# Two first batches of a linear-attention block written straight into place, with their bonus sums on TensorE and their state update deferred

## The reference

```python
# attention: batch 4, heads 8, sequence 768, head_dim 48, all fp32
for t in range(S):
    cur = einsum('bhd,bhe->bhde', u[None] * k[t], v[t])
    y[t] = einsum('bhd,bhde->bhe', r[t], state + cur)
    state = w[None, :, :, None] * state + einsum('bhd,bhe->bhde', k[t], v[t])
x = y as [3072 tokens, 384]
# first MLP (384 -> 2048 -> 384)
h = x @ w_in;  g = h * sigmoid(1.702 * h);   x = g @ w_out
# second MLP, its own weights
h = x @ w_in2; g = h * tanh(softplus(h));    out = g @ w_out2
```

## Time and profile before

| what | value |
|---|---|
| median of 3 runs | 919.5 us (919.02 to 2286.22) |
| the profiled execution's own time | 920.33 us |
| its span, first to last instruction | 918.4 us |
| mean granted TensorE clock | 0.987 |
| PE busy | 896.6 us (98%) |
| DVE, ACT, POOL busy | 335.4, 290.4, 178.9 us |

### The profile page before, as it was taken

One profiled execution on the slowest core, in us unless ns is written; L12 is line 12 of the kernel. 1 busy time (PEld: TensorE's weight loads), 2 busy tenths in 40 slices (PEclk: granted clock), 3 DMA queues, 4 the chain that ended last, 5 costly groups with the idle time before them and its releaser, 6 DMA issues.

```text
span 918.4 us, 12827 instructions
## 1 busy us (share of the span) xinstructions
PE 896.6 (98%) x5126; PEld 748.9 (82%) x5126; DVE 335.4 (37%) x465; ACT 290.4 (32%) x526; POOL 178.9 (19%) x145
## 2 busy tenths in 40 slices
PE   7797999999999999999999999999999999999998
PEld 7697888888888888888888888888888888888886
DVE  6474744543443454335145322122121221222211
ACT  1353223223222322322245532332323322322332
POOL 5585850432325043222000000000000000000000
PEclk9798999999999999999999999999999999999999
DMA  9755320321132032112412000000000000000000
GB/s 212 168 113 115 76 67 16 81 52 45 48 82 61 14 82 52 45 48 51 142 53 86 0 1 0 35 1 1 35 0 1 35 1 1 35 0 1 35 1 34
DMA packets 33289, 44.28 MB, mean 48 GB/s; under 512 B 5712, under 2 KB 27856, under 8 KB 33232
## 3 DMA queue, kind: packets, MB, share of 16 engines
q1 hardware_dynamic: 31312, 42.24, 17.3%
q10 hardware_dynamic: 1920, 1.23, 0.6%
HBM read 36.37 MB, written 4.72 MB: 45 GB/s over the span
## 4 chain that ended last, share of the span: by engine, by line
PE 90%; SPq 4%; DMA 2%; issue 1%; POOL 1%; DVE 1%; ACT 1%; POOLq 0%; DVEq 0%; ACTq 0%
PE h L879 42%; PE acc L906 41%; PE y_bank L821 2%; PE a_bank L805 2%; PE y_bank L833 2%; SPq L337 2%; SPq L333 1%; DMA mid<-in_wts 1%; DMA xs<-xs 1%; PE a_bank L846 1%; POOL win_lo L442 1%; SPq L311 0%; PE y_bank L919 0%; PE acc L919 0%; DMA arena<-in_rk 0%
## 5 line engine op out<-in xcount | busy, mean ns | idle before, releaser
L716 DVE TENSOR_TENSOR g_lo<-act,g_hi 128x512 fp32r<-128x512 f32 (+1 forms) x201 | 180.7, 900 | 512.0 <-ACT g_hi L546 511.8
L879 PE MATMUL h<-xs,win_hi 128*128 128x512 f32 (+1 forms) x1206 | 342.2, 387 | 7.6 <-ACT g_hi L546 3.1
L879 PEld LDWEIGHTS h<-xs,win_hi 128*128 128x128 f32 x1206 | 221.9, 191 | 53.6 <-POOL win_lo L442 5.6
L543 ACT ACTIVATE act<-h 128x512 f32<-128x512 f32 (+1 forms) x201 | 116.3, 578 | 274.2 <-PE h L879 274.0
L546 ACT ACTIVATE g_hi<-h 128x512 fp32r<-128x512 f32 (+1 forms) x201 | 116.4, 579 | 255.5 <-PE acc L906 255.4
L906 PE MATMUL acc<-g_hi,wout_hi 128*128 128x512 f32 (+1 forms) x603 | 168.1, 381 | 0.0
L906 PE MATMUL acc<-g_hi,wout_lo 128*128 128x512 f32 (+1 forms) x603 | 168.1, 381 | 0.0
L906 PE MATMUL acc<-g_lo,wout_hi 128*128 128x512 f32 (+1 forms) x603 | 168.0, 381 | 0.0
L879 PE MATMUL h<-xs,win_lo 128*128 128x512 f32 (+1 forms) x603 | 165.6, 383 | 0.0
L879 PEld LDWEIGHTS h<-xs,win_lo 128*128 128x128 f32 x603 | 112.4, 191 | 22.0
L906 PEld LDWEIGHTS acc<-g_hi,wout_hi 128*128 128x128 f32 x603 | 111.6, 189 | 21.6
(11 more groups left out here) (76 smaller groups left out, 421.6 us busy)
## 6 DMA issues: line engine op xcount, KB each, us to landing
arena<-in_rk SPq DMA_DIRECT2D x48, 192.0 KB, 3.5
arena<-in_wts SPq DMA_DIRECT2D x16, 384.0 KB, 3.6
arena<-in_r SPq DMA_DIRECT2D x24, 192.0 KB, 3.8
arena<-in_k SPq DMA_DIRECT2D x22, 192.0 KB, 3.6
arena<-in_v SPq DMA_DIRECT2D x22, 192.0 KB, 3.7
out<-mid SPq DMA_DIRECT2D x5, 768.0 KB, 3.3
xs<-xs SPq DMA_DIRECT2D x141, 16.0 KB, 1.8
mid<-in_wts SPq DMA_DIRECT2D x1, 1152.0 KB, 7.1
```

Of the source, the lines that this page charges most:

```text
L543: act.activation(act1[:, g % 2, 0:c1 - c0], h_bank[g % 2][:, 0:c1 - c0], GATES[layer])
L716: dve.tensor_tensor(g_lo[:, g % 2, cols], act1[:, g % 2, cols], f32(g_hi[:, g % 2, cols]), ALU.subtract).then_inc(glo_done, 1)
L879: ins = pe.matmul(hb, w[:, f, kd, :], x_part(lo, par, kd)[:, c0:c1], start=i + kd == 0, stop=i == 2 and kd == KD - 1)
```

## The change

For the first two batches the two heads of the fourth pair are no longer moved. A copy of their v, split in three pieces of 16 columns each behind 48 columns of zeros (`vs_pad`), is multiplied with their scores over 64 rows, so that the 16-row pieces come out in the rows where the moves would have put them; the other six heads are added on top. The bonus sums of these two batches are made on PE (`early_sums`: the elementwise product of the decayed r and k, times u/w in a small table `pick` loaded one value at a time), so `rr`, the bonus steps and the first reduction fall away for them. Their `ks` are loaded later, and their state update is put at step `LATE` = 8 of the stream. POOL decays `rk` of batch 1 in place of DVE, DVE makes two `low_out`, the loads are put in another order, `HALF` becomes 10, `scores(2)` moves from ahead of the stream into its step 0, and three of the six moves of batch 3 go from SP's queue to ACT's.

```diff
-HALF = 9
+HALF = 10
+LATE = 8
-SCORES = [{2: 3, 8: 4, 12: 5, 15: 6, 18: 7}] + ...
-BURST = [{1: 2, 4: 3, 11: 4, 14: 5, 17: 6, 20: 7}] + ...
+SCORES = [{0: 2, 3: 3, 9: 4, 12: 5, 16: 6, 19: 7}] + ...
+BURST = [{2: 2, 5: 3, 11: 4, 14: 5, 18: 6, 21: 7}] + ...
# SP
-            for n in range(2):
+            for n in range(EARLY):
                 sp.wait_ge(rk_clear, n + 1)
                 load_rk(n)
-                load_kv(n)
-                load_rr(n)
...
+            for n in range(EARLY):
+                load_v(n)
+            sp.wait_ge(cleared, 2)
+            for j, p0 in enumerate((0, ODD)):
+                sp.dma_start(pick[p0:p0 + D, :, j], u_d.rearrange("o (h a d) -> d (o h) a", h=HP, a=2)[:, :, j],
+                             allow_slow_non_contiguous=True).then_inc(pick_in, 16)
+            load_k(2)
+            load_rr(2)
+            for i, (to, rows, landed) in enumerate(pieces):        # group 1
+                if i == 6:
+                    sp.wait_ge(a_done, 2)
+                    sp.wait_ge(prod_done, 1)
+                    load_rk(2)
+                    load_v(2)
                     sp.dma_start(bonus_u, u_d.broadcast_to([P, DM])).then_inc(u_in, 16)
+                sp.dma_start(to, rows).then_inc(landed, 16)
             sp.wait_ge(a_done, 4)
+            sp.wait_ge(prod_done, 2)
             load_rk(3)
+            load_k(3)
             load_rr(3)
-            move_x(0)
-            move_x(1, half=True)
+            sp.wait_ge(dtrn, 1)
             load_group(2)
-            load_again(B)
+            load_v(3)
+            for n in range(EARLY):
+                load_k(n)
             move_x(2)
-            move_x(3)
-            load_again(B + 1)
+            for n in range(B, B + 2):
+                sp.wait_ge(y_done, n - 1)
+                load_rk(n)
+                load_rest(n)
+            move_x(3, half=True)
...
             load_group(3)
             for n in range(B, NT * B):
+                if n + 2 < NT * B:
+                    sp.wait_ge(y_done, n + 1)
+                    load_rk(n + 2)
                 move_x(n)
                 if n + 2 < NT * B:
-                    load_again(n + 2)
+                    load_rest(n + 2)
# GpSimd
+            pool.wait_ge(w_in, 32)
+            pool.wait_ge(pick_in, 32)
+            pool.tensor_tensor(pick, pick, powers[:, 0, 0, :]...broadcast_to([PR_ROWS, HP, 2]), ALU.mult)
             pool.wait_ge(runs, 2 * LOGS)
+            pool.wait_ge(rk_in[1], 32)
+            pool.tensor_tensor(first[1].rk, first[1].rk, decay, ALU.mult).then_inc(r_dec, 1)
+            for n in range(EARLY):
+                product(n)
...
-            for n in range(EARLY):
-                bonus(n)
-            pool.wait_ge(dtab, 1)
-            for n in range(EARLY):
-                decay_k(n)
# ScalarE, ahead of the stream
-            act.wait_ge(kv_in[0], 32)
+            act.wait_ge(rk_in[0], 32)
...
+            for n in range(EARLY):
+                act.wait_ge(v_in[n], 16)
+                act.activation(vs_pad[n][:, :, :, D:ODD], first[n].vs[:, H - 2:H, :]..., ACT.Copy).then_inc(padded, 1)
# ScalarE, in the stream, ahead of the step's split_in and split_out
                     attention(t, s)
+                    if t == 0 and s == LATE:
+                        for n in range(EARLY):
+                            first_state(n)
+                    if t == 0 and s in BURST[t] and BURST[t][s] == B - 1:
+                        act.wait_ge(xlo_done, B)
+                        for i, (to, rows) in enumerate(x_pieces(B - 1)):
+                            if i >= KD:
+                                act.dma_start(to, rows).then_inc(moved[B - 1], 16)
# VectorE, ahead of the stream
             select(0)
-            decay_rk(1)
+            select(1)
             diagonal(0)
-            select(1)
             diagonal(1)
             x_lo_part(0)
             x_lo_part(1)
             decay_rk(2)
-            select(2)
-            diagonal(2)
+            low_out(0)
+            low_out(1)
# TensorE
+                if n < EARLY:                                       # inside(n)
+                    pe.wait_ge(padded, EARLY + n + 1)
+                    for kd in range(KD):
+                        for half, p0 in enumerate((0, ODD)):
+                            pe.matmul(y_of(n)[p0:p0 + ODD, kd * CH:(kd + 1) * CH], vs_pad[n][:, half, kd, :], e.amat[:, half, HP - 1, :],
+                                      start=kd == 0, stop=False, skip_group_check=True)
+                    (six more for heads 0 to 5)
+            def early_sums(n):
+                pe.wait_ge(pick_done, 1)
+                pe.wait_ge(prod_done, n + 1)
+                for hp in range(HP):
+                    ins = pe.matmul(early_dots[n]...[:, hp, :], rk_prod[n][:, hp, :], pick[:, hp, :], start=True, stop=True)
+                if t == 0 and s == LATE:                            # attention(t, s)
+                    pe.wait_ge(state_new, 2 * (B - EARLY))
+                    for n in range(EARLY):
+                        update(n)
             scores(0)
-            decay_rows()
-            keep_warm(early_bank, 6)
-            scores(1)
-            keep_warm(early_bank, 2)
-            inside(0)
-            keep_warm(early_bank, 8)
-            inside(1)
-            update(0)
-            update(1)
-            pe.wait_ge(dtab, 1)
-            keep_warm(decay_bank, 4)
-            scores(2)
-            keep_warm(decay_bank, 8)
+            keep_warm(early_bank, 2)
+            scores(1)
+            early_sums(0)
+            keep_warm(early_bank, 2)
+            early_sums(1)
+            inside(0)
+            keep_warm(early_bank, 2)
+            inside(1)
+            decay_rows()
+            keep_warm(early_bank, 8)
```

More of the change, by code:

```diff
@@ L107, in mlp_rwkv_program @@
         LOGS = CH.bit_length()
+        pick = part(2 * HP)[0:PR_ROWS, :].rearrange("p (h a) -> p h a", h=HP)
         powers = part(LOGS * 2 * HP)[0:PR_ROWS, :].rearrange("p (n s h) -> p n s h", n=LOGS, s=2)
@@ L132, in first_operands, with borrow @@
             return e
+        unused = [(SLOTS - 3) * 2 * DM]
+        def borrow(cols):
+            unused[0] += cols
+            assert unused[0] <= SLOTS * 2 * DM
+            return mid[:, unused[0] - cols:unused[0]]
+        rk_prod = [borrow(HP * CH)[0:PR_ROWS, :].rearrange("p (h t) -> p h t", h=HP) for _ in range(EARLY)]
+        decay_t = borrow(HP * CH)[0:PR_ROWS, :].rearrange("p (h t) -> p h t", h=HP)
+        vs_pad = [borrow(DM).rearrange("p (a k e) -> p a k e", a=2, k=KD) for _ in range(EARLY)]
         later = [operands(b) for b in range(B)]
@@ L151, in mlp_rwkv_program @@
         early_bank = acc[1]
+        early_dots = [bank[:, 0:H] for bank in (y_bank, acc[0])]
         w_in = sem("w_in")
@@ L156, in mlp_rwkv_program @@
         rk_in = [sem(f"rk_in{b}") for b in range(B)]
-        kv_in = [sem(f"kv_in{b}") for b in range(B)]
+        k_in = [sem(f"k_in{b}") for b in range(B)]
+        k_first = [sem(f"k_first{b}") for b in range(EARLY)]
+        v_in = [sem(f"v_in{b}") for b in range(B)]
+        padded = sem("padded")
+        pick_in = sem("pick_in")
+        pick_done = sem("pick_done")
+        prod_done = sem("prod_done")
+        early_done = sem("early_done")
         rr_in = [sem(f"rr_in{b}") for b in range(B)]
@@ L470, in _ @@
                 low_out(f)
+            pool.wait_ge(dtab, 2)
             def low(f0, f1):
@@ L577, in _ @@
             split_out(0, 0)
+            split_out(0, 1)
             split_in(0, 2)
-            act.wait_ge(xlo_done, 2)
-            for i, (to, rows) in enumerate(x_pieces(1)):
-                if i >= KD:
-                    act.dma_start(to, rows).then_inc(moved[1], 16)
-            split_out(0, 1)
-            act.wait_ge(cleared, 2)
-            for n in range(EARLY):
-                first_state(n)
+            act.wait_ge(dtrn, 1)
+            for a, d0 in enumerate((0, ODD)):
+                act.activation(decay_s.rearrange("p (h a d) -> p h a d", h=HP, a=2)[:, :, a],
+                               decay_bank[:, 0:HP * PR_ROWS].rearrange("p (h d) -> p h d", h=HP)[:, :, d0:d0 + D], ACT.Copy).then_inc(dtab, 1)
+            act.wait_ge(cleared, 3)
             gate(0, 0)
@@ L758, in tile @@
                         split_g(g + 1)
-                    if t == 0 and s == 0:
+                    attention(t, s)
+                    if t == 0 and s == 1:
                         decay_rk(3)
-                        dve.wait_ge(dtab, 1)
+                        dve.wait_ge(dtab, 2)
                         decay_k(2)
-                    attention(t, s)
-                    if t == 0 and s == 2:
+                    if t == 0 and s == 4:
                         decay_k(3)
+                    if t == 0 and s == LATE - 1:
+                        for n in range(EARLY):
+                            decay_k(n)
                     if switch:
@@ L848, in update @@
                 ins.then_inc(ds_done, 1)
```

(7 more changed lines are left out.)

198 lines of the change are left out of this document (115 added, 83 removed).

## The result

The median is 908.06 us (907.63 to 909.12, 4 runs) against 919.26 for the kernel before beside it: a ratio of 0.9885, with an interval of 0.9865 to 0.9904. The gain, 1.15%, is clear of the noise and smaller than the 2% that the forecast asked for to call the kernel faster; the forecast's median was 900.6. The profiled execution took 908.21 us, 12.1 less than the one before; 18.9 were forecast.

The account below looks back on a forecast made before the run. PE was taken as busy after 141.64 us, so only the stretch before counted: 33.9 us ahead of the stream, 17.4 lost inside it. Terms summed to -18.9 us, giving 900.6 us; own range 896 to 904, 892 to 910 for 8 in 10.

Parts of the forecast that it names:

- first rival: Prologue slower than worked out: clock falls ahead of `inside(0)`, or `pick` lands late; +3 to +6 us, 905; chance 0.21.
- The new start, -11.8: Ahead of the stream: without moves, tile 0's first `up` comes at 22.1 us, not 33.86, 11.8 us sooner.
- late weights: Rival at the start: weight group 0 lands at 21.70 again, start 23.8, groups 1 and 2 late; 905; chance 0.07.
- slow `pick`: Rival at the start: `pick`'s 384 values served one after another; 909, or 921 and up; chance 0.04.
- The clock at the start: PE's prologue and stream start: clock taken as kept through shorter holes, -2.3 us; if it falls, start some 3.5 later.
- Work inside the stream, +2.6: Tile 0's stream on PE: `scores(2)` 1.28, two late updates 1.1 and the tenth block in halves 0.24 add 2.6 us.
- group 3, -7.8: Weight group 3, issued sooner by SP: ACT's wait, PE's two stalls and the half clock behind them go, 7.8 us less.
- The small waits, -0.5: PE's waits for POOL's `low_in` in the stream: 1.9 us for 2.4, 0.5 us less.
- ACT's moves, +2.2 and +1.9: Step 5: batch 3's moves delay `split_in(8)` and the next step's `up`, +2.2 us; half clock behind the idle time, +1.9.
- The state of piece 5, -3.2: `scores(6)`: `rk` n+2 loaded ahead of the moves of n removes PE's state wait and half clock, 3.2 us less.
- Next late is the same weight group, with two steps of slack on PE: Said of weight group 3: once its wait is gone, the next late thing is that group again, covered by two steps.
- The rival that the moves cost little: DVE or POOL slack swallows ACT's moves of batch 3, or the clock stays up: -4.1 us, 896.5; chance 0.18.

Follow-up runs that it names:

- experiment 6: Changed kernel with all six moves of batch 3 issued by SP, none by ACT: 909.62 us, ratio 0.9884 to the kernel before.
- experiment 8: Changed kernel with low remainders of weight blocks 10 to 15 set to zero by POOL's memset, not subtracted: 906.28 us, ratio 0.9854 to the kernel before.
- experiment 10: Changed kernel with the load of `rk` n+2 behind the moves of n again: 910.9 us, ratio 0.9895 to the kernel before.
- experiment 1: Changed kernel with POOL's wait for `pick` and its product behind the decay of batch 1's `rk`: 907.02 us, ratio 0.9854 to the kernel before.
- experiment 2: Changed kernel with five more `keep_warm` behind `scores(0)` and four ahead of `inside(0)`: 905.68 us, ratio 0.9852 to the kernel before.
- experiment 3: As experiment 2, plus one unused 128-column matmul between each two two-column matmuls of `early_sums`: 908.05 us, ratio 0.9875 to the kernel before.
- experiment 7: Changed kernel with `decay_k(2)` ahead of `decay_rk(3)` on DVE: 908.22 us, ratio 0.9874 to the kernel before.
- experiment 5: Changed kernel with ACT's three moves of batch 3 issued behind the step's splits: 910.0 us, ratio 0.9886 to the kernel before.
- experiment 11: Changed kernel with experiments 2 and 5, and `scores(7)` and the bursts of 5 and 6 one step later: 902.82 us, ratio 0.9817.
- experiment 9: Changed kernel with `select` and `diagonal` ahead of `g_lo` on DVE at tile 0's later steps with `scores`: 909.58 us, ratio 0.9891 to the kernel before.
- experiment 12: Changed kernel with experiments 1, 3 (fewer added warmings) and 5, the steps of experiment 11, late `decay_k` one step sooner: 899.64 us, ratio 0.9795.

## Why the prediction was right or wrong

Right: the direction, and the range (892 to 910, measured 908.06). Too large: the size, 18.9 us for 12.1; the forecast's own narrower range, 896 to 904, was missed. That the wide range held is partly luck: the first rival accounts for 2.6 of the 6.7 us between the two sums, and the other large part, 3.5, is in no rival. The sign "first `up` after 25 us" was missed by 0.4 us, and three of the six other kernels with this prologue show it. Point by point:

- **The new start, -11.8.** `pick`, the weights and `scores(1)` came as worked out, so neither the late weights nor the slow `pick` happened. What failed is the step "*The clock at the start* ... I take it as kept": it kept for the stream (so -2.3 holds) but not for the prologue, where 7 us at half clock cost the start 2.5 (0.7 to 4.2 in the seven kernels with this prologue). That is the first rival. Its reason was half of it: it and the forecast both looked at the holes of PE, and the hole ahead of `scores(1)` does precede the fall in experiments 6, 8 and 10. But experiments 1 and 2 closed the holes to 0.3 to 0.4 us without keeping the clock, and experiment 3 shows that the two-column `early_sums` then bring it down. They had been priced by their time alone (0.5 us).
- **Work inside the stream, +2.6, and group 3, -7.8:** as forecast; the splits that had waited wait 0.31 us in all.
- **The small waits, -0.5, measured +0.7.** The step put the meeting of `decay_rk(3)` with `low_in(4)` on PE's wait for POOL. The wait is on the other side, DVE's `decay_k(2)` behind `decay_rk(3)`, 1.30 us; experiment 7 shows that either order leaves one of the two late.
- **ACT's moves, +2.2 and +1.9:** right in place and size, 2.2 and 1.6. Experiment 5 shows the cause, and also that the loss isn't saved by removing it alone.
- **The state of piece 5, -3.2:** measured -3.5.
- **The missing term, +3.5.** The step that failed is "Next late is the same weight group, with two steps of slack on PE", said of group 3, and with it the step on piece 5, which asked of the sooner loads only what POOL and the state gain. Next late was DVE. PE's stall for group 3 and POOL's pauses had been DVE's time (read from the two timelines; no run puts them back as they were); with them gone or short `g_lo` took 3 us and more beside POOL, and `inside` waited for `diagonal` three times. Experiment 8 shows that POOL's subtractions are behind 0.99 and 1.90 of it, experiment 11 that a step more for DVE ends it. The mechanism was in the earlier trace rows, where `low_in` took 2.42 us; the forecast applied it to step 1 alone.

The rival that the moves cost little didn't happen.

**What stays open.** Which part of the load order takes POOL's pauses, and how much of the 2.9 us is due to POOL's reads rather than to the length of its work. Each term comes from single profiled executions, while the ratios of most experiments overlap: that 1, 2 and 8 are each ahead of the change by some 0.3% isn't settled. Nor is it what decides whether a fall of the clock follows an idle time: behind 2.5 us it did in seven kernels and not in experiment 2, behind the last wait for `diagonal` (1.9 to 1.95 us) it did in experiments 1 and 7 and not in the kernel after.

## What to carry to other kernels

An engine's idle time on a shared resource is another engine's working time: when a load is moved so that one engine no longer waits, look at what its neighbour got done in that pause. Where several waits lie a fraction of a microsecond behind each other, a single repair measures nothing (experiments 5 to 7, 9 and 10 all lie within 0.2% of the change), and only together are they worth their sum (experiments 11 and 12); so after each removed wait ask who is late next, and mend the row of them. Work moved to TensorE in very narrow matmuls is priced by what it does to the clock as well as by its length. And before a cause is read from one trace, look at the same stretch in every kernel that shares it: here seven traces of one prologue showed a fall at three different places.

## What the runs showed of the hardware that was not expected

- Two groups of four two-column matmuls (fp32, so 16 records) are followed by a fall of the granted clock though PE shows as busy: 0.58 over 3.50 us with PE busy for 3.50 (experiment 2), and 1.00 over 4.00 us with a 128-column one between each two (experiment 3).
- A hole of 1.20 to 1.67 us behind `scores(0)` was followed by a fall within `scores(1)` in three kernels, one of 0.96 to 1.17 us in four was not; the falls there came later, at 14 to 16 us.
- The element-wise load of `pick`, 384 values of 4 bytes in two transfers, landed 4.2 us after its issue, and the 192 KB load of v issued just ahead took 4.5. Transfers at work from 3 to 12 us in the kernel after (operation, count, KB each, median us to landing):

```profile
mid<-in_v SPq DMA_DIRECT2D x2, 192.0 KB, 4.5
arena<-in_u SPq DMA_DIRECT2D x2, 0.8 KB, 4.2
```

  So at this size its shape cost nothing that the full queues don't explain. That each value has a descriptor of its own, as the Trainium skill has it (DMA: Bandwidth & Descriptors, Rules for kernel authors), is neither borne out nor denied by a time.
- DVE's masked copy, the last step of `diagonal`, varies as `g_lo` does. It took 3.23 us in this row of the kernel after, begun 0.35 us into a POOL multiplication of 2.41 us, but 1.31 in the earlier trace rows, also with POOL at work beside it (16.44 to 19.45 us), so POOL's presence alone doesn't decide it:

```profile
63.68 3.23 DVE L765 COPY_PREDICATED arena<-arena 128x1024 f32<-128x1024 uint32 x1
```
